# Heads 1 to 4 prepared by ScalarE, row maxima in runs: another order for the opening of an attention and MoE kernel

## What is computed

```python
# attention: batch 2, 8 heads, 768 tokens, head width 64; 16 clusters per head
q_assign = argmax(einsum('bhsd,hcd->bhsc', q_n, c_n), -1)   # q_n, k_n, c_n: rows over their norms
k_assign = argmax(einsum('bhsd,hcd->bhsc', k_n, c_n), -1)
mask = q_assign[:, :, :, None] == k_assign[:, :, None, :]
scores = where(mask, scale * q @ k.T, -1e9)
scores = scores - max(scores, -1)
attn = exp(scores); attn = attn / (sum(attn, -1) + 1e-9)
x = attn @ v
# mixture of experts: 1536 tokens, 512 wide, 8 experts, top 1, relu, width 1024
# feed-forward: ((x @ w_a) * (x @ w_b)) @ w_out, width 1536
```

## Time and profile before

| | us |
|---|---|
| median of 3 executions | 854.85 |
| the three | 852.8, 854.85, 854.87 |
| profiled execution | 858.68 |
| its span | 856.8 |
| first scores of head 0 (start of round 0) | 38.06 |
| first scores of head 1 (start of round 1) | 66.29 |

### The profile page before, as it was taken

How to read it: one execution, slowest core, us unless ns; L and a number is a source line. 1 busy time by engine, 2 the same in 40 slices (tenths; PEclk the granted TensorE clock), 3 DMA queues, 4 the chain that set the end, 5 groups by cost and what they waited for, 6 DMA issues and landing times.

```text
span 856.8 us, 13231 instructions
## 1 busy us (share of the span) xinstructions
PE 815.2 (95%) x5451; PEld 739.1 (86%) x5451; DVE 423.0 (49%) x696; ACT 285.3 (33%) x497; POOL 120.7 (14%) x111
## 2 busy tenths in 40 slices
PE   5989999999999999579999999999999999999996
PEld 4779999999999999469999999988888888888885
DVE  6667776667777652567555555634213111221111
ACT  3212333333233343445555555533213111211111
POOL 1002211112221010113333330000001000010001
PEclk9989999999999999679999999999999999999998
DMA  4312222222222243077777667530001000010001
GB/s 122 82 44 70 68 57 52 61 59 54 66 72 50 56 145 114 18 242 221 214 200 215 200 199 238 181 124 1 1 0 50 1 1 0 1 50 1 0 1 49
DMA packets 58239, 72.37 MB, mean 84 GB/s; under 512 B 17800, under 2 KB 40192, under 8 KB 58176
## 3 DMA queue, kind: packets, MB, share of 16 engines
q1 hardware_dynamic: 54944, 63.71, 25.6%
q0 software_dynamic: 2784, 7.58, 2.9%
q10 hardware_dynamic: 448, 0.19, 0.1%
HBM read 57.24 MB, written 6.30 MB: 74 GB/s over the span
## 4 chain that ended last, share of the span: by engine, by line
PE 90%; DVE 4%; DMA 2%; issue 2%; POOL 1%; ACT 0%; SPq 0%; POOLq 0%; ACTq 0%; DVEq 0%
PE bank L1394 14%; PE bank L1638 8%; PE bank L1639 8%; PE bank L1640 8%; PE pair L1348 5%; PE pair L1597 3%; PE pair L1599 3%; PE pair L1598 3%; PE bank L1317 3%; PE bank L1325 2%; PE first_pair L1378 2%; PE first_pair L1380 2%; PE first_pair L1657 2%; PE first_pair L1658 2%; PE first_pair L1656 2%; PE bank L1657 2%
## 5 line engine op out<-in xcount | busy, mean ns | idle before, releaser
L1394 PE MATMUL bank<-v_sb,prob 128*128 128x104 f32 x1152 | 144.8, 276 | 0.0
L1394 PEld LDWEIGHTS bank<-v_sb,prob 128*128 128x128 f32 x1152 | 140.5, 193 | 0.2
L960 DVE TENSOR_REDUCE neg_max<-pair 128x1 f32<-128x768 f32 x93 | 88.7, 954 | 67.1 <-PE pair L1348 67.1
L1265 DVE TENSOR_TENSOR g_sb<-bank,a_sb 128x512 f32<-128x512 f32 x36 | 24.9, 691 | 187.5 <-PE bank L1640 187.5
L1638 PE MATMUL bank<-x_hi,wt 128*128 128x512 f32 x288 | 112.1, 389 | 1.7 <-issue 1.7
L1640 PE MATMUL bank<-x_hi,wt 128*128 128x512 f32 x288 | 112.1, 389 | 0.0
L1639 PE MATMUL bank<-x_lo,wt 128*128 128x512 f32 x288 | 112.0, 389 | 0.0
L682 ACT ACTIVATE prob<-first_pair 128x384 f32<-128x384 f32 x128 | 59.2, 490 | 132.4 <-PE first_pair L1380 132.4
L1027 DVE TENSOR_TENSOR wt<-w_raw,wt 128x2048 fp32r<-128x2048 f32 x41 | 93.6, 2287 | 15.7 <-ACT wt L717 15.7
L717 ACT ACTIVATE wt<-w_raw 128x2048 fp32r<-128x2048 f32 x41 | 78.2, 1909 | 0.5 <-issue 0.5
L1597 PE MATMUL pair<-ht_hi,wt 128*128 128x240 f32 x256 | 71.3, 279 | 0.0
(11 more groups left out here) (244 smaller groups left out, 1602.3 us busy)
## 6 DMA issues: line engine op xcount, KB each, us to landing
w_raw<-in_moe_w_dram SPq DMA_DIRECT2D x32, 1024.0 KB, 7.8
q_raw<-in_q_dram SPq DMA_DIRECT2D x16, 192.0 KB, 2.4
k_raw<-in_k_dram SPq DMA_DIRECT2D x16, 192.0 KB, 2.5
v_sb<-in_v_dram SPq DMA_DIRECT2D x16, 192.0 KB, 3.0
qb<-qa SPq DMA_DIRECT2D x16, 192.0 KB, 2.6
kc<-kd SPq DMA_DIRECT2D x16, 192.0 KB, 2.6
w_raw<-in_moe_w_a_dram SPq DMA_DIRECT2D x3, 1024.0 KB, 5.3
w_raw<-in_moe_w_b_dram SPq DMA_DIRECT2D x3, 1024.0 KB, 8.1
```

The source lines that it names most:

```text
L960: dve.tensor_reduce(neg_max[n % 2][:, t:t + 1], masked_in(n, t)[:, :, 0:HALF], AX.XY, ALU.max, negate=True).then_inc(mx_done, 1)
L1394: last = pe.matmul(o_ps[:, t * VW:t * VW + VZ], prob[s][:, j, t * P:(t + 1) * P], v_in_sb[u][:, j, :], start=(j == 0 and t == 0), stop=(j ...
```

## The change

ScalarE, not VectorE, now makes the high parts of heads 1 to 4 and all four operand copies of head 3. TensorE's order changes: the turning of the one-hot rows of heads 0 and 1 comes earlier, between other heads' transposes; one masked tile of head 1 stands ahead of round 0; the logits of head 2 move from the prologue into round 0; there are nine `keep_busy` matmuls in place of ten. VectorE reduces rows in longer runs, sums v for head 0 ahead of the maxima, makes two constants earlier and a third (`upper_bf`) in round 1. On SyncE's queue `load(3)` goes ahead of `operands(1)` and `load(4)` behind `operands(2)`. Rounds 1 to 15 keep their order.

```diff
@@ SyncE @@
             load_v(1)
+            load(3)
             operands(1)
             hot_rows(0)
-            load(3)
-            load(4)
             load_v(2)
-            operands(2)
             row_max(0)
             hot_rows(1)
+            operands(2)
+            load(4)
@@ ScalarE @@
+            def high_parts(n):
+                s = n % 2
+                act.wait_ge(qk_in[s], 32 * (n // 2 + 1))
...
+                act.activation(q_split[s][:, :, 0:D], q_raw[s][:].rearrange("p (t d) -> p t d", t=NT),
+                               ACT.Copy).then_inc(hi_ready, 1)
+                act.activation(k_split[s][:, :, D:2 * D], k_raw[s][:].rearrange("p (t d) -> p t d", t=NT),
+                               ACT.Copy).then_inc(hi_ready, 1)
             first_unit(0)
             first_unit(2)
-            for n in (1, 2):
-                for unit in range(4):
-                    unit0(n, unit)
+            act.wait_ge(hi_ready, 2)
+            high_parts(1)
+            for unit in range(4):
+                unit0(1, unit)
+            high_parts(2)
+            for unit in range(3):
+                unit0(2, unit)
             row_max(0)
-            for r in range(HEADS):
+            unit0(2, 3)
+            high_parts(3)
+
+            exps(0, 0)
+            exps(0, 1)
+            exps(0, 2)
+            high_parts(4)
+            exps(0, 3)
+            unit0(3, 0)
+            exps(0, 4)
+            row_max(1)
+            unit0(3, 1)
+            v_means(0)
+            unit0(3, 2)
+            exps(0, 5)
+            unit0(3, 3)
@@ VectorE @@
             centroids_out()
+            dve.wait_ge(cst_in, 16)
+            dve.tensor_copy(ident_bf[:], ident)
+            dve.tensor_copy(desc_bf[:], cst[:, C_D16:C_D16 + C])
             first_unit(1)
             centroids_in()
             first_unit(3)
-            high_parts(1)
...
-            high_parts(2)
             logits_maxed(0)
             one_hot(0)
             mask_rows(0)
             find_keys(0)
+            sum_v(0)
+            logits_maxed(1)
+            one_hot(1)
             for t in range(NT):
                 row_max(0, t)
...
+            for t in range(4):
+                row_max(2, t)
             logits_maxed(3)
             one_hot(3)
+            row_max(2, 4)
             token_major(0)
@@ TensorE @@
-            for unit in range(4):
-                unit0(1, unit)
+            unit0(1, 0)
+            unit0(1, 1)
             unit0(0, 5)
+            unit0(1, 2)
+            unit0(1, 3)
             unit0(0, 6)
             unit0(1, 4)
             masked_scores(0, 0)
             masked_scores(0, 1)
...
+            unit0(1, 5)
...
             unit1("max", 0)
+            keep_busy(3)
+            unit0(1, 6)
+            unit0(2, 3)
             keep_busy(6)
+            masked_scores(1, 0)
             scores_t(0, 0)
             scores_t(0, 1)
             times_v(0, 0)
+            masked_scores(1, 1)
+            unit0(2, 4)
             scores_t(0, 2)
+            masked_scores(1, 2)
+            times_v(0, 1)
+            masked_scores(1, 3)
...
+            masked_scores(2, 4)
+            times_v(0, 5)
             masked_scores(2, 5)
-            times_v(0, 5)
```

More of the change, by code:

```diff
@@ L722, in first_unit @@
                                ACT.Copy).then_inc(first_act, 1)
+            def high_parts(n):
+                s = n % 2
+                act.wait_ge(qk_in[s], 32 * (n // 2 + 1))
+                if n == 2:
+                    act.wait_ge(first_full, 4)
+                elif n > 2:
+                    full, base = operand_bank(n - 2)[1::2]
+                    act.wait_ge(full, base + 4)
+                act.activation(q_split[s][:, :, 0:D], q_raw[s][:].rearrange("p (t d) -> p t d", t=NT),
+                               ACT.Copy).then_inc(hi_ready, 1)
+                act.activation(k_split[s][:, :, D:2 * D], k_raw[s][:].rearrange("p (t d) -> p t d", t=NT),
+                               ACT.Copy).then_inc(hi_ready, 1)
             first_unit(0)
             first_unit(2)
-            for n in (1, 2):
-                for unit in range(4):
-                    unit0(n, unit)
-            row_max(0)
-            for r in range(HEADS):
+            act.wait_ge(hi_ready, 2)
[5 more added lines that the diff above has]
+                unit0(2, unit)
+            row_max(0)
+            unit0(2, 3)
[13 more added lines that the diff above has]
+            unit0(3, 3)
+            for r in range(1, HEADS):
                 if r == HEADS - 2:
@@ L737, in _ @@
                 exps(r, 2)
-                if r >= 1 and valid(r + 1): row_max(r + 1)
+                if valid(r + 1): row_max(r + 1)
                 for t in early_square(r, 0): square(t, junk)
@@ L741, in _ @@
                 exps(r, 3)
[L742 to L744 removed]
                 for n in made(r): unit0(n, 2)
                 for t in early_square(r, 1): square(t, junk)
[L747 removed]
+                exps(r, 4)
                 v_means(r)
@@ L863, in high_parts @@
                 s = n % 2
+                if n == 5:
+                    dve.wait_ge(hi_ready, 10)
                 dve.wait_ge(qk_in[s], 32 * (n // 2 + 1))
[L865 to L869, removed]
+                full, base = operand_bank(n - 2)[1::2]
+                dve.wait_ge(full, base + 4)
                 dve.tensor_copy(q_split[s][:, :, 0:D],
@@ L1080, in _ @@
                     experts_out()
+                    dve.tensor_copy(upper_bf[:], cst[:, C_UP:C_UP + P])
                 if r == 2:
@@ L1445, in _ @@
             masked_scores(0, 1)
[L1446 to L1449, removed]
+            unit0(1, 5)
+            masked_scores(0, 2)
+            masked_scores(0, 3)
+            unit0(2, 0)
+            masked_scores(0, 4)
+            unit0(2, 1)
+            masked_scores(0, 5)
+            unit0(2, 2)
             unit1("max", 0)
-            unit0(2, 4, 1)
+            keep_busy(3)
+            unit0(1, 6)
+            unit0(2, 3)
             keep_busy(6)
[L1453 to L1456, removed]
+            masked_scores(1, 0)
             scores_t(0, 0)
@@ L1460, in _ @@
             times_v(0, 0)
-            masked_scores(1, 0)
+            masked_scores(1, 1)
+            unit0(2, 4)
             scores_t(0, 2)
-            masked_scores(1, 1)
+            masked_scores(1, 2)
+            times_v(0, 1)
+            masked_scores(1, 3)
             unit0(2, 5)
-            times_v(0, 1)
-            masked_scores(1, 2)
+            scores_t(0, 3)
+            masked_scores(1, 4)
+            times_v(0, 2)
             unit0(2, 6)
[L1468 to L1472, removed]
             masked_scores(1, 5)
             scores_t(0, 4)
-            masked_scores(2, 0)
+            unit0(3, 0)
+            unit1("max", 1)
             unit0(3, 1)
-            unit1("max", 1)
-            masked_scores(2, 1)
-            unit0(3, 2)
             unit1("mean", 0)
             times_v(0, 3)
+            unit0(3, 2)
+            masked_scores(2, 0)
+            scores_t(0, 5)
+            unit0(3, 3)
+            masked_scores(2, 1)
+            times_v(0, 4)
             masked_scores(2, 2)
-            unit0(3, 3)
-            scores_t(0, 5)
+            unit0(3, 4, 0)
             masked_scores(2, 3)
-            unit0(3, 4)
+            unit0(3, 4, 1)
             masked_scores(2, 4)
-            times_v(0, 4)
+            times_v(0, 5)
             masked_scores(2, 5)
-            times_v(0, 5)
             for r in range(1, HEADS):
```

20 lines of the change are left out of this document (4 added, 16 removed).

## The result

| | median us | lowest to highest | executions |
|---|---|---|---|
| before | 854.75 | 852.8 to 854.87 | 4 |
| changed | 861.19 | 860.12 to 862.52 | 4 |

The ratio is 1.0069 [1.0046, 1.0092]: slower, by 6.4 us in the medians, where 2.5 us less had been forecast. (A ratio here is worked out from all executions of both kernels, with its 95% interval, so it need not be that of the two medians.) The profiled executions took 861.90 (span 860.0) and 858.68 (span 856.8) us, 3.2 apart. How much of the 6.4 belongs to the change is a question of its own; the last experiment bears on it.

The account below looks back on a forecast made before the run. TensorE, busy 95% of the span, bounds the kernel, so the start of round 1 decides: 36.3 + 27.5 = 63.8 us against 66.29, a gain of 2.5, 854.85 - 2.5 = 852.35 us; range 850.6 to 857.0.

Parts of the forecast that it names:

- Each step of the opening: Ahead of round 0: first masked tile at 22.4 us instead of 22.93, round 0 at 36.3, 1.8 earlier.
- ScalarE's high parts: Opening and round 0: high parts moved to ScalarE take 0.5 us each; cost on the path taken as 0.
- The second of the two DMAs that had to land: Ahead of round 0: head 1's hot rows land at 35.7 us, just when needed; 0.3 late at most.
- The wait ahead of head 1's fourth masked tile: Round 0: TensorE waits 1.6 us for a maximum that GpSimd's subtraction delays by holding the one-hot's last step.
- the length of round 0: Round 0: 21.4 us of work, 5.7 of waits and 0.4 left out by the walk, 27.5 against 28.2 before.
- All of it supposes that the clock stays up in round 0: Round 0: the forecast case, full clock and waits as walked, 851.3 to 853.5 us, chance 0.42.
- it falls twice, and the second time into round 1: Rival, rounds 0 and 1: two falls, the second at head 2's last masked tile, 858.1 us, chance 0.14.
- The fall of before: Round 0 of before: 6.8 us at half clock cost 3.1 to 3.4 us, which the change would save.
- 1.2 of waits, 0.4, 1.0 of work: Round 0 losses: waits 5.7 for 4.5, 0.4 left out by the walk, head 2's logits in, a masked tile out.

Follow-up runs that it names:

- the last experiment: The changed kernel run again, unaltered, ten executions: 856.33 us against 855.02 for before, ratio 1.0019.
- all fillers: Changed kernel plus 35 matmuls of 64 columns, result unread, in TensorE's waits of round 0: 860.04 us against 856.34 for before, ratio 1.0045.
- wide fillers: Changed kernel plus six and five matmuls of 512 columns in its two long waits: 853.56 us against 855.02 for before, ratio 0.9997.

## Why the prediction was wrong

**What held.** Each step of the opening, within 0.4 us up to the first masked tile and 1.0 us early at round 0 (35.33 for 36.3). ScalarE's high parts: 0.51 and 0.52 us, 0.5 taken. The second of the two DMAs that had to land is tight, as forecast: the changed kernel's first trace shows no wait for it, its second one 0.94 us, with round 0 at 35.17 all the same:

```profile
34.71 0.62 PE L1369 MATMUL pair<-kc,qb 80*128 80x384 f32 x2 [0.94 <-DMA kc<-hot_t]
```

The wait ahead of head 1's fourth masked tile, 1.52 for 1.6, and its cause: `hot`, with two inputs, is held beside GpSimd's subtraction, 0.97 for 0.36, while the reduction of 0.94 behind it, beside GpSimd's second subtraction, is not. That agrees with the Trainium skill, SBUF — State Buffer, "Who interferes with whom", by which a VectorE instruction with two SBUF inputs contends with GpSimd's reads and a reduction never does. Even the length of round 0 held where the clock was kept up: 27.6 us in the three traces with all fillers or wide ones, 27.5 in the sum.

**The step that failed.** "All of it supposes that the clock stays up in round 0" (0.42). It did not: 23.9 us between rounds 0 and 2 ran at half clock, against the 6.8 of before, and cost 8.8 us. The rival "it falls twice, and the second time into round 1" (0.14) is what both traces of the changed kernel show. The first fall is where it was looked for, behind the 1.52 us wait. The second is not: the rival put it behind a wait of 1.2 us ahead of head 2's last tile, and it began 2.8 us before that tile, behind two waits of 0.47 us. The sum had a row against it: the one wait as long as the 1.6 forecast, 1.46 us in before, was followed by 0.50, and it was set against rows that showed no fall behind shorter waits. In the six traces that have such a wait (1.46 to 1.52 us) the clock fell in five; the sixth is before with the 35 matmuls behind attention. A forecast at full clock should not have been the likeliest case, and a fall was not certain either.

**The size of the rival was off too.** It priced two falls of 6.8 us at 2.4 and 3.4, together 5.8 us, 858.1 in all. Measured between rounds 0 and 2, against the 46.4 us with the clock up: 8.8 us in the first trace, with 13.7 and 10.2 us at half clock, and 5.3 in the second, with 3.4 and 10.2. So the second trace cost about what the rival said, with other lengths, and that agreement is luck. The 23.5 us that TensorE was busy at half clock in the first would by themselves be 11.7 us of lost work; the measured loss is smaller, presumably because slow matmuls shorten the waits. The fall of before was over-priced as well, 3.1 to 3.4 us for a measured 2.5.

**What the order is worth with the clock up.** Within the fast sort of opening the changed kernel starts round 2 at 80.62 and 80.73 and before at 81.93: 1.2 to 1.3 us for the reordering, in single traces. It starts round 0 2.9 us earlier, and rounds 0 and 1 take 1.7 us longer. The forecast had 1.8 for the first, and 2.6 more in round 0 (1.2 of waits, 0.4, 1.0 of work): by its own terms the order lost 0.8, and its whole gain of 2.5 was the fall of before that would go. A fall that before does not have in every execution, and costs 2.5 us where it does, cannot carry that.

**The range.** It ended at 857.0 for a two-falls case worked out at 858.1, and treated the 2.1 us of three runs as the spread. Before's own executions went from 852.4 to 859.6 on the three chips of the experiments. That alone asked for a wider upper end.

**What is shown and what stays open.** Shown: with the clock held, by three different sets of added matmuls in four kernels, rounds 0 and 1 take 8.8 to 9.0 us less than in the first trace of the changed kernel, so the falls are what that trace lost; the rival theory of an order that is slower by itself is out, as round 2 then starts before that of the kernel before. Shown as well: in the median the change is slower, by 0.7% in four executions and by 0.2%, with an interval that touches 1, in ten later ones on another chip. Open: how large it is in truth; what decides whether a wait of 1.5 us is followed by a fall, and whether that lasts 3.4 us or 17.1; and why the opening comes in two sorts. The traces with falls of different length are single executions, and no run here separates the chip from the draw.

## What to carry to other kernels

Where TensorE is saturated but for a few waits, look at the longest waits that a change leaves and not only at their sum: behind one of 1.5 us the clock was halved for 3 to 17 us in five traces of six, and that cost more than the wait. A row of before that shows such a fall belongs in the forecast as a likely case. Before crediting an order with a gain, fill the long waits of both kernels with matmuls that nobody reads and compare those, from a point that lies behind what varies by itself (here the start of round 0). One trace of each kernel is not enough for that. And look at the later stages of every kernel to which instructions were added: a stop with the releaser "issue" that comes and goes with their number is not the edit's.

## What was not expected of the hardware

- The clock fell behind waits of 1.17 to 1.52 us with TensorE busy for 1.76 to 2.25 of the 3.4 or 3.5 us around them, behind waits of at most 0.47 us in four traces, and once with 3.48 of 3.50 us busy. It stayed up behind a wait of 1.47 us in an unaltered attention (1.60 of 3.40 us busy), and behind waits of 0.47 us in the kernel with wide fillers. The low stretches lasted 3.4, 6.8, 10.2, 13.7 or 17.1 us, one kernel's own two traces differing, with TensorE busy for 13.23 of 13.60 us in one of them.
- The same opening ran with head 0's logits in 1.48 us or in 2.71 us, and round 0 started 0.9 to 1.7 us earlier with the first.
- 35 matmuls of 16 columns in idle time stopped TensorE for 4.13 us eight matmuls into a later stage, and a fall of 3.4 us followed: 862.16 against 855.89. With the 70 instructions of the fillers the stop came nine matmuls in and took 3.51 us; with 40 instructions more on top of these 70 there is none.
- Executions of before on one chip differ by 5 to 7 us (852.4 to 859.6 over three chips), those of the changed kernel by 6.5 (854.2 to 860.7). Four executions gave an interval for the changed kernel ([1.0046, 1.0092]) that ten later ones did not confirm ([0.9999, 1.0039]).
